# Prefix counts of the routing in attention, taken as two halves of 64 rows

## What is computed

```python
def _attn_ref(u, v, z):                      # u, v: 4 x 2496 x 256, z: 4 x 2496 x 64
    scores = (1.0 / S) * np.matmul(z, z.transpose(0, 2, 1))
    attn = np.maximum(scores, 0.0) ** 2
    return u * np.matmul(attn, v)

def _moe_ref(x, w_skip, w_gate, w1, w2):     # rows with x @ w_skip > 0 are computed, others pass
    e_idx = np.argmax(xc @ w_gate, axis=1)   # one expert of 8 for each row
    y[mask] = gate_w[mask, None] * (np.maximum(xc[mask] @ w1[e], 0.0) @ w2[e])
    out[do_compute] = xc + y
...
def _moe2_ref(x, modality_id, w_gate, modality_bias, w1, w2):
    logits = x @ w_gate + modality_bias[modality_id]   # then as above, for every row
```

## Time and profile before

| what | value |
|---|---|
| time, median of 3 runs | 1489.77 us (1489.64 to 1490.29) |
| time of the profiled execution | 1489.09 us |
| its span, from first to last instruction | 1487.2 us |
| mean granted TensorE clock | 0.996 of full speed |
| PE busy | 1464.6 us, 98% of the span |
| DVE busy | 1009.1 us, 68% |
| ACT busy | 779.3 us, 52% |
| POOL busy | 399.2 us, 27% |
| share of PE in the chain that ended last | 95% |

### The profile page before, as it was taken

One profiled execution on the slowest core, in us unless ns is written; L12 is line 12 of the kernel. 1 busy time (PEld: TensorE's weight loads), 2 busy tenths in 40 slices (PEclk: granted clock), 3 DMA queues, 4 the chain that ended last, 5 costly groups with the idle time before them and its releaser, 6 DMA issues.

```text
span 1487.2 us, 34548 instructions
## 1 busy us (share of the span) xinstructions
PE 1464.6 (98%) x11853; PEld 1279.1 (86%) x11853; DVE 1009.1 (68%) x2377; ACT 779.3 (52%) x1542; POOL 399.2 (27%) x379
## 2 busy tenths in 40 slices
PE   8999999999999999999899999999999999999997
PEld 7888988888888898888899999998888888888885
DVE  7989987999889998987666666665333343333332
ACT  6677766777667766765344444444333333333332
POOL 4133322334224332323222222224121221211212
PEclk9999999999999999999999999999999999999999
DMA  5311030211302020021533354322211121111110
GB/s 121 100 40 56 29 101 29 66 43 53 92 31 66 29 87 29 30 87 65 180 104 127 121 192 133 106 97 94 90 44 44 43 69 46 43 44 43 58 44 26
DMA packets 58009, 107.74 MB, mean 72 GB/s; under 512 B 18007, under 2 KB 32354, under 8 KB 57884
## 3 DMA queue, kind: packets, MB, share of 16 engines
q0 software_dynamic: 18464, 58.68, 11.3%
q1 hardware_dynamic: 39420, 47.48, 11.1%
HBM read 75.63 MB, written 32.04 MB: 72 GB/s over the span
## 4 chain that ended last, share of the span: by engine, by line
PE 95%; DMA 1%; issue 1%; DVE 1%; POOL 0%; SPq 0%; ACT 0%; POOLq 0%; ACTq 0%; DVEq 0%
PE pO L1480 33%; PE pS L1737 11%; PE pO L1745 10%; PE pS L1469 9%; PE pO L1680 9%; PE pS L1697 9%; PE pO L1747 5%; PE pM L1737 4%; PE pT L1728 1%; PE pO L1489 1%; PE pT L1627 1%; PE pM L1547 1%; PE pT L1532 1%; PE pO L1609 1%; DMA raw<-in_v_dram 0%
## 5 line engine op out<-in xcount | busy, mean ns | idle before, releaser
L1120 DVE TENSOR_TENSOR AL<-A,AH 128x512 fp32r<-128x512 f32 (+1 forms) x400 | 313.5, 784 | 13.7
L1480 PE MATMUL pO<-AH,VH 64*128 64x512 f32 (+1 forms) x1520 | 297.9, 383 | 2.6 <-POOL VL L555 1.3
L1480 PE MATMUL pO<-AL,VH 64*128 64x512 f32 (+1 forms) x1520 | 297.2, 382 | 0.0
L1480 PE MATMUL pO<-AH,VL 64*128 64x512 f32 (+1 forms) x1520 | 296.8, 381 | 0.0
L725 ACT ACTIVATE R<-pS 128x512 f32<-128x512 f32 (+1 forms) x400 | 213.4, 588 | 157.7 <-PE pS L1469 157.4
L734 ACT ACTIVATE A<-R 128x512 f32<-128x512 f32 (+1 forms) x400 | 229.7, 624 | 11.1 <-DVE AL L1120 10.9
L1118 DVE CAST AH<-A 128x512 fp32r<-128x512 f32 (+1 forms) x400 | 212.9, 532 | 30.9 <-ACT A L734 30.6
L1745 PE MATMUL pO<-VL,AH 128*128 128x512 f32 x640 | 232.2, 400 | 0.0
L1378 DVE SCALAR_TENSOR_TENSOR AL<-pS,AH 128x512 fp32r<-128x512 f32 x120 | 83.0, 692 | 157.2 <-ACT AH L896 157.1
L1747 PE MATMUL pO<-VL,AL 128*128 128x256 f32 x640 | 179.2, 280 | 0.0
L609 POOL DMA_INDIRECT out_dram<-xrow,tok_at x80 | 77.8, 973 | 365.4 <-DVE xrow L1388 352.9
(11 more groups left out here) (249 smaller groups left out, 2493.6 us busy)
## 6 DMA issues: line engine op xcount, KB each, us to landing
raw<-in_w_dram POOLq DMA_DIRECT2D x22, 1024.0 KB, 7.7
A<-token_rows SPq DMA_DIRECT2D x21, 536.0 KB, 3.5
uT<-in_u_dram SPq DMA_DIRECT2D x16, 512.0 KB, 3.7
xin<-token_rows SPq DMA_DIRECT2D x24, 268.0 KB, 3.0
raw<-in_v_dram SPq DMA_DIRECT2D x4, 1152.0 KB, 5.8
A<-in_w2t_dram POOLq DMA_DIRECT2D x8, 512.0 KB, 4.8
raw<-in_v_dram SPq DMA_DIRECT2D x4, 768.0 KB, 7.3
raw<-in_z_dram SPq DMA_DIRECT2D x8, 368.0 KB, 5.0
```

Source lines behind the costliest of these rows:

```text
L1120: v_.tensor_tensor(AL[k % NBUF][:, 0:n], A[k % NA][:, 0:n], AH[k % NBUF][:, 0:n].bitcast(F32), ALU.subtract).then_inc(al_ready, 1)
L1480: last = t_.matmul(pO[:, (KD * r + d) * QW:(KD * r + d) * QW + n], vv[rows, vo + k * D + d * P:vo + k * D + (d + 1) * P], a[k % NBUF][rows ...
```

## The change

In attention (`idx < CHUNKS`, the routed chunks 1 to 19) the ten matmuls of `prefixes` take half of the rows each: those over rows 0 to 63 write to columns 256 to 335 of `pT`, those over rows 64 to 127 to the same columns of `pM`. DVE adds the halves: `rank` takes `base` and the first half, then the second; `base` too is added to twice. `rank` and `base` thus have one more step each, and `ROUTE` goes from 15 to 17. Behind attention (chunk 20) the counts are made as before, with two step numbers left unused.

```diff
-ROUTE = 15
+ROUTE = 17
...
+        prefix_halves = [x[:, 2 * P:2 * P + (QT + 1) * GR].rearrange("p (t n) -> p t n", n=GR) for x in (pT, pM)]
...
-                step(v_.tensor_tensor(rank[:, :, :], prefix[:, 0:QT, :], base[:, None, :].to_broadcast([P, QT, GR]), ALU.add))
-                v_.tensor_tensor(base[:, :], prefix[:, QT, :], base[:, :], ALU.add).then_inc(base_ready, 1)
+                parts = prefix_halves if idx < CHUNKS else [prefix]
+                step(v_.tensor_tensor(rank[:, :, :], parts[0][:, 0:QT, :], base[:, None, :].to_broadcast([P, QT, GR]), ALU.add))
+                if idx < CHUNKS:
+                    step(v_.tensor_tensor(base[:, :], parts[0][:, QT, :], base[:, :], ALU.add))
+                    step(v_.tensor_tensor(rank[:, :, :], parts[1][:, 0:QT, :], rank[:, :, :], ALU.add))
+                v_.tensor_tensor(base[:, :], parts[-1][:, QT, :], base[:, :], ALU.add).then_inc(base_ready, 1)
...
-                t_.matmul(pM[:, 2 * P:2 * P + (QT + 1) * GR], before[:, :], oh[:, :, :].rearrange("p t g -> p (t g)"), start=True, stop=False)
+                whole = [(prefix, slice(0, P))]
+                parts = list(zip(prefix_halves, halves)) if idx < CHUNKS else whole
+                for to, rows in parts:
+                    t_.matmul(to, before[rows, :], oh[rows, :, :], start=True, stop=False)
                 for i in range(QT):
-                    last = t_.matmul(prefix[:, i + 1:QT + 1, :], ones[:, :], oh[:, i:i + 1, :].to_broadcast([P, QT - i, GR]),
-                                     start=False, stop=(i == QT - 1))
+                    for to, rows in parts:
+                        last = t_.matmul(to[:, i + 1:QT + 1, :], ones[rows, :], oh[rows, i:i + 1, :].to_broadcast([P // len(parts), QT - i, GR]),
+                                         start=False, stop=(i == QT - 1))
```

## The result

The change makes the kernel slower by 0.2%: 3.2 us by the medians, 1.8 to 4.0 by the interval.

What follows compares the result with a forecast made beforehand. PE alone was taken to set the pace in attention; 18 × 0.19 = 3.4 us saved there less 0.37 lost at its end made 3.05, so 1489.77 − 3.05 = 1486.7 us, range 1485.5 to 1489.3.

Steps and rivals of the forecast that it cites:

- So this costs nothing in routed chunks 1 to 18: DVE's added 0.46 us per routed chunk is covered: smallest lead at the tiles 1.6 us, DVE idle 71 of 640 us.
- Nothing else comes late in its place: In attention, PE asking 0.2 us earlier finds its tiles ready, so the 3.4 us saved is not lost to other waits.
- no idle time of PE before L1485: Sign of success in attention: PE never idles before its sums of A times V.
- the tiles stay ahead of PE: Sign of success in attention: DVE's split tiles still ready over 1 us before PE takes them.
- The waits between the modes: Around the counts on PE, switching between 64 and 128 rows: 0.15 becomes 0.06, 0.10 becomes 0, 0.19 us saved per chunk.
- the load of 0.11: Load of the scores' weights behind the counts on PE, uncovered, forecast to stay at 0.11 us.
- Ten half counts in pairs: Prefix counts on PE: halves start together and pairs keep today's pace, 0.13 us for all; forecast's chance 0.60.
- the rival with the Trainium skill's figure: Half counts on PE take turns, 60 cycles each: nine steps 0.22 us, saving 0.10 per chunk; turns' chance 0.12.
- The stretch: PE from the last transposes at p == 7 through the counts to the scores' second pair: 0.30 us instead of 0.49.
- DVE's two steps: The added additions for rank and base on DVE: 0.25 and 0.21, together 0.46 us per routed chunk.
- The end of attention: Chain from chunk 19's counts to xin: counts 0.09 earlier, dest 0.46 later, 0.37 us lost, bounds −0.1 to +0.8.
- The slower rival: Counts on PE: halves in turn, each with its own load, 0.22 more per chunk, 1494.5 us; chance 0.07.

Runs made afterwards that it cites:

- e1: Kernel before plus DVE's two extra additions, into a spare tile, in routed chunks 1 to 19, PE's counts left whole: 1494.45 us against 1490.18, ratio 1.0031.
- e10: Kernel before plus DVE's two extra steps only in routed chunks 4, 5, 9, 10 and 14 to 18: 1490.36 us against 1491.13, ratio 0.9997.
- e11: Changed kernel with base fused as fifth block of rank and the step adding 1e-9 to the gates' denominator left out: 1487.14 us against 1491.13 before.
- e3: Changed kernel with DVE's first pO sum two tiles earlier in the nine chunks that wait: 1503.48 us against 1490.18 for the kernel before.
- e6: Changed kernel with DVE's first pO sum one tile earlier in the nine chunks that wait: 1494.05 us against 1490.32 for the kernel before.
- e4: Control: kernel before with DVE's first pO sum two tiles earlier in the same nine chunks: 1502.32 us against 1490.18.
- e7: Control: kernel before with DVE's first pO sum one tile earlier in the same nine chunks: 1493.58 us against 1490.32.
- e8: Changed kernel with half counts and DVE's two steps only in routed chunks 4, 5, 9, 10 and 14 to 18: 1487.77 us against 1490.32 before.
- e2: Kernel before plus DVE's two extra steps done twice, four in each routed chunk, counts whole: 1501.59 us against 1491.13, ratio 1.0072.

## Why the prediction was wrong

**The failed step: "So this costs nothing in routed chunks 1 to 18".** I took DVE's leads at the tiles, found 1.6 us at the least, and stopped. DVE makes a second thing that PE waits for, the sums of `pO`, and there the slack was about 0.33 us in six chunks and none in three (5, 10, 15). The 71 us that DVE is idle said nothing, since they lie elsewhere. e1 shows the price of that step, 4.3 us; e10 shows that it is owed to nine chunks alone.

**"Nothing else comes late in its place"** failed with it: what PE gained at the counts of those chunks it spent waiting. The sign that I had named, no idle time of PE before L1485, failed nine times; that the tiles stay ahead of PE told nothing about the sums.

**The waits between the modes**: right. 0.15 became 0.06, 0.10 became 0 and the load of 0.11 stayed.

**Ten half counts in pairs**: right, 0.12 from the first pair to the last for the 0.13 I took, with the fast load kept. The overhead of each matmul that the rival with the Trainium skill's figure put in a row does not add up across two halves that run side by side. The stretch is 0.29 for 0.30, the saving 0.2 for 0.19, and 18 × 0.2 is 3.6 for 3.4. No run has this gain by itself: in e11, the nearest, the medians give 4.0 us (2.4 to 5.1) and attention 2.1, since the tight chunks keep next to nothing of it.

**DVE's two steps**: the size was right, 0.47 for 0.46. The cost of the meetings with POOL that they shift was missing: 0.38 us ahead of chunk 3.

**The end of attention**: forecast 0.37 lost, in this execution 0.25 gained (15.66 for 15.91). `dest` came late as I said, but POOL's four scatters, which I bounded with some tenths, took less: from the first one's issue to the last one's 4.14 us (706.00 to 710.14) for 4.70 (702.42 to 707.12). Pieces of the chain of waits after the change, start, duration, what:

```profile
703.42 0.24 DVE rank L1093
...
706.00 0.36 POOL token_rows L549
...
710.14 2.62 DMA token_rows<-xkeep,dest
```

From `rank` to the last landing's start are 6.72 us (703.42 to 710.14) where there were 6.82, though `rank` to `dest` is 0.46 longer. It is no chance of one execution: the stretch "to `xin`" takes 15.66 to 15.78 in the four versions with these two steps and no fused `base` (after, e1, e3, e6), and 15.91 to 16.21 in the five with DVE's steps there as before (before, e4, e7, e8, e10). In e2, with four steps, it is 16.82, so it goes both ways.

**The rivals.** None was this one. The slower rival had 0.07 and stood on PE, at halves that follow each other; they don't, and that its 1494.5 us lies near the measured time is luck. I looked for the loss where the change was made and not at the engine that paid for it. The sum by the right step, with the stalls read from the trace of after: 3.6 us gained, less the stalls at nine chunk starts. From the intervals above, (0.85 + 0.20) twice and 0.10 + 0.20 for the first group of three chunks, and as much for the other two, are 7.2 us: 3.6 net lost, and 3.8 measured.

**What stays open.** The meetings with POOL were seen and sized in the traces but no run was made to take them away by themselves. How the loss splits between the steps and the meetings is shown ahead of chunk 3 (0.27 and 0.38) and, by the one meeting in e1 that went the other way, ahead of chunk 13 (0.45 and 0.39, there without PE's 0.20). Why chunks 5, 10 and 15 lose only 0.1 to 0.2 I have not followed, nor what PE waits for in e2's gate columns.

## What to carry to other kernels

When an edit adds work to an engine that is not the bound, list everything that the bounding engine takes from it, not only the most frequent product, and take the smallest slack over that list, chunk by chunk. Then spend the added work only in the iterations that have room: the same edit in nine chunks out of nineteen gained 2.5 us, and in all of them it lost 3.2. And before moving one step of an engine ahead, look at whom it releases; a neighbour that starts sooner can collide with the steps that follow, as POOL's multiply did in e7.

## What the runs showed of the hardware

- A GpSimd `tensor_tensor` of 128x512 (1.30 us) stops a DVE subtract of two SBUF operands, 0.69 us to 1.66 to 1.82, and a DVE cast of 0.42 us lasted 5.68 beside four of them. Which of the two pays hung on the order of their starts, within 0.02 us (e1): with DVE first, its subtract kept 0.69 us and POOL's took 1.82. A shift of some tenths of a us moves what it hits, so the price of an added step on DVE isn't its duration.
- bf16 matmuls on the two halves of the rows start together, and the pairs stand 0.02 to 0.04 us apart for 80 to 16 columns, with loads of 0.09 to 0.10 us each; the pair costs no more than one on all rows.
- Going between matmuls on half the rows and on all cost 0.09 us on the way in and 0.10 on the way out, and both were gone when all stayed on halves.
